# Probabilities times values grouped by head, at slots 2, 5, 8 and 11 of the pair loop

## What is computed

```python
mask = q_bucket[:, :, :, None] == k_bucket[:, :, None, :]
scores = scale * np.matmul(q, k.transpose(0, 1, 3, 2))
scores = np.where(mask, scores, -1000000000.0)
scores = scores - np.max(scores, axis=-1, keepdims=True)
attn = np.exp(scores)
attn = attn / (np.sum(attn, axis=-1, keepdims=True) + 1e-09)
return np.matmul(attn, v).astype(np.float32)
...
X = np.fft.fft(x, axis=1)
X = np.fft.fft(X, axis=2)
```

## Time and profile before

| | us |
|---|---|
| median of three runs | 653.95 (653.85 to 654.36) |
| the profiled execution | 655.48, of which its span 653.7 |
| PE busy in the span | 624.0 |
| VectorE, ScalarE, GpSimd busy | 351.7, 314.6, 245.6 |
| one pair in the loop | 30.01 |

### The profile page before, as it was taken

The page is one execution under the profiler, slowest core; times in us unless marked ns, Lnnn a source line. Parts: engine busy times, 40 slices in busy tenths (PEclk is TensorE's granted clock), DMA queues, the critical chain, the costliest instruction groups (busy, mean ns, idle before and its releaser), DMA issues.

```text
span 653.7 us, 11131 instructions
## 1 busy us (share of the span) xinstructions
PE 624.0 (95%) x3730; PEld 503.3 (77%) x3730; DVE 351.7 (54%) x587; ACT 314.6 (48%) x608; POOL 245.6 (38%) x199
## 2 busy tenths in 40 slices
PE   2899999999999999888999999999999999999998
PEld 1667676667667675887788888888888888888786
DVE  2878797868787785987211111114533333329920
ACT  2777686768686764364422222225333333354242
POOL 6543333333252340845332223334644444313140
PEclk9999999999999999999999999999999999999999
DMA  5822231313242000100122222341212222000102
GB/s 129 249 80 72 73 95 50 96 51 99 70 116 73 1 26 1 50 0 1 34 66 64 64 64 64 121 136 33 71 58 64 64 64 65 16 0 1 76 21 97
DMA packets 34262, 42.08 MB, mean 64 GB/s; under 512 B 3520, under 2 KB 22208, under 8 KB 34240
## 3 DMA queue, kind: packets, MB, share of 16 engines
q1 hardware_dynamic: 32512, 37.77, 19.5%
q0 software_dynamic: 1728, 4.02, 2.2%
HBM read 38.63 MB, written 3.15 MB: 64 GB/s over the span
## 4 chain that ended last, share of the span: by engine, by line
PE 81%; DVE 10%; issue 4%; ACT 2%; POOL 2%; DMA 1%; SPq 0%; ACTq 0%; DVEq 0%; POOLq 0%
PE banks L1487 21%; PE banks L1475 20%; PE banks L1302 10%; PE banks L1285 10%; PE banks L1349 7%; PE banks L1582 4%; DVE row_min L953 2%; PE banks L1241 2%; PE banks L1566 2%; PE banks L1422 2%; DVE x_then_u_then_gate L1160 1%; DVE probT L341 1%; DVE k_b L946 1%; PE banks L1325 1%; POOL row_sums_and_differences L523 1%
## 5 line engine op out<-in xcount | busy, mean ns | idle before, releaser
L1147 DVE SCALAR_TENSOR_TENSOR h_lo<-banks,h_hi 128x512 fp32r<-128x512 f32 x64 | 35.3, 557 | 181.3 <-ACT h_hi L808 181.3
L953 DVE TENSOR_REDUCE row_min<-banks 128x1 f32<-128x768 f32 x96 | 91.2, 955 | 42.2 <-PE banks L1285 41.7
L660 ACT ACTIVATE prob<-banks,row_min 128x768 f32<-128x768 f32 x96 | 87.1, 907 | 31.1 <-DVE row_min L953 31.1
L1475 PE MATMUL banks<-unT_hi,w_hi 128*128 128x512 f32 (+1 forms) x256 | 86.5, 338 | 0.2 <-DVE h_lo L1147 0.2
L1475 PE MATMUL banks<-unT_hi,w_lo 128*128 128x512 f32 (+1 forms) x256 | 86.3, 337 | 0.0
L1475 PE MATMUL banks<-unT_lo,w_hi 128*128 128x512 f32 (+1 forms) x256 | 86.2, 337 | 0.0
L1349 PE MATMUL banks<-ident,prob 128*128 128x128 f32 x576 | 79.6, 273 | 2.4 <-DVE probT L341 1.5
L546 POOL TENSOR_TENSOR w_lo<-w_stage,w_hi 128x512 fp32r<-128x512 f32 x32 | 45.3, 1416 | 80.0 <-ACT w_hi L725 80.0
L484 POOL TENSOR_TENSOR k_b<-k_raw,k_a 64x768 fp32r<-64x768 f32 x16 | 29.1, 1820 | 122.1 <-ACT k_a L643 122.1
L1349 PEld LDWEIGHTS banks<-ident,prob 128*128 128x128 f32 x576 | 67.3, 140 | 9.8 <-ACT probT L341 2.6
L551 POOL TENSOR_TENSOR w_lo<-w_stage,w_hi 128x512 fp32r<-128x512 f32 x32 | 42.2, 1318 | 75.5 <-ACT w_hi L730 75.5
(11 more groups left out here) (147 smaller groups left out, 1192.3 us busy)
## 6 DMA issues: line engine op xcount, KB each, us to landing
w_stage<-in_moe_w_ch SPq DMA_DIRECT2D x64, 256.0 KB, 2.8
q_raw<-in_q SPq DMA_DIRECT2D x32, 192.0 KB, 3.2
k_raw<-in_k SPq DMA_DIRECT2D x32, 192.0 KB, 3.6
v_in<-in_v SPq DMA_DIRECT2D x16, 192.0 KB, 2.4
out<-y_out SPq DMA_DIRECT2D x12, 256.0 KB, 2.0
seq_tables_sb<-in_dft POOLq DMA_DIRECT2D x6, 386.0 KB, 3.5
wvo_stage<-in_moe_w_val SPq DMA_DIRECT2D x1, 1024.0 KB, 5.3
wvo_stage<-in_moe_w_out SPq DMA_DIRECT2D x1, 1024.0 KB, 7.7
```

The source lines that it names most:

```text
L660: act.activation(prob[s % 2][:, :, :], s_tile(s), ACT.Exp, bias=row_min[:, s:s + 1], scale=-1.0, accum_out=row_sum[:, s:s + 1]).then_inc(e ...
L953: dve.tensor_reduce(row_min[:, s:s + 1], s_tile(s), AX.XY, ALU.min).then_inc(min_ready, 1)
L1147: dve.scalar_tensor_tensor(out=h_lo[:, slot, at:at + size], in0=h_bank[c], scalar=0.0, in1=h_hi[:, slot, at:at + size].bitcast(F32), op0=A ...
L1475: op = pe.matmul(h_bank[c], w_[:, slot, kb, :], x_[:, kb, at:at + size], start=(kb == 0 and m == 0), stop=(kb == KB - 1 and m == 2))
```

## The change

The products are grouped by head instead of by half of the queries: a result bank now holds one head, its first 384 queries on partitions 0 to 63 and the others on 64 to 127, and both column halves of PE hold that head's values. Head 0 is multiplied in slots 8 and 11 of its own pair, head 1 in slots 2 and 5 of the next. O moves from slots 3 and 6 to 3 and 9, B from 1 and 7 to 0 and 6. The outT copies go before the exponential of slots 1 and 7, and `round_q` with `copy_q` after that of slots 2 and 8. The values are loaded head by head with a semaphore each. The inverted row sums are held per head, and `write_x` writes 64 columns of all six row tiles instead of 128 columns of three. The first roundings of the folded rows move from slots 0 and 2 to 2 and 3 of pair 8. Pair 1 is written out too, and the loops cover pairs 2 to 6.

```diff
-        PREPARE = {1: ["B"], 2: ["C0"], 4: ["C1"], 7: ["B"], 8: ["C0"], 10: ["C1"]}
+        PREPARE = {0: ["B"], 2: ["C0"], 4: ["C1"], 6: ["B"], 8: ["C0"], 10: ["C1"]}
...
-        OUT_SLOT = {3: 0, 6: 1}
+        OUT_SLOT = {3: 0, 9: 1}
...
-        PV_SLOTS = {11: (0, 0), 1: (0, 1), 2: (1, 0), 4: (1, 1)}
+        PV_PARTS = 2
+        PV_SLOTS = {8: (0, 0, 0), 11: (0, 0, 1), 2: (1, 1, 0), 5: (1, 1, 1)}
...
-            def load_v(i):
-
-                need(sp, pv_done, 2 * i)
-                for h in range(2):
-                    sp.dma_start(v_in[:, h, :, :], v_v[2 * i + h]).then_inc(v_loaded, 16)
+            def load_v(i, h):
+
+                need(sp, pv_done, 2 * i + (h - 1) if not isinstance(i, int) or i else 0)
+                sp.dma_start(v_in[:, h, :, :], v_v[2 * i + h]).then_inc(v_loaded[h], 16)
...
-                    if last == 2 and s in (0, 2):
-                        round_parts(0, s // 2)
                     h, nxt = head_of(s)
                     if s % 6 == 0 and last + nxt < 2:
                         round_k(i + nxt, h)
+                    if s % 6 == 1 and not (isinstance(i, int) and i == 0):
+                        copy_outT(i, s // 6)
                     if last < 2:
                         softmax_exp(i, s)
-                    if s % 6 == 0 and last + nxt < 2:
+                    if s % 6 == 2 and last + nxt < 2:
                         round_q(i + nxt, h)
-                    if s % 6 == 1 and last + nxt < 2:
                         copy_q(i + nxt, h)
-                    if s == 1 and not (isinstance(i, int) and i == 0):
-                        copy_outT(i, 0)
-                    if s == 4 and not (isinstance(i, int) and i == 0):
-                        copy_outT(i, 1)
+                    if last == 2 and s in (2, 3):
+                        round_parts(0, s - 2)
...
-                for kt in range(HT * part, HT * part + HT):
-                    for h in range(2):
-                        op = pe.matmul(PS[h * D:(h + 1) * D, 7, 0:HALF], v_in[:, h, kt, :],
+                for kt in range(T // PV_PARTS * part, T // PV_PARTS * (part + 1)):
+                    for g in range(2):
+                        op = pe.matmul(PS[g * D:(g + 1) * D, 7, 0:HALF], v_in[:, h, kt, :],
                                        probT[h][:, kt, g * HALF:(g + 1) * HALF], start=(kt == 0), stop=(kt == T - 1))
...
-                    if s == 10 and last < 2:
+                    if s == 8 and last < 2:
                         invert_sums(i, 0)
-                    if s == 1 and not first:
+                    if s == 2 and not first:
                         invert_sums(i - 1, 1)
```

More of the change, by code:

```diff
@@ L174, in attention_fft_ffn_gate_kernel @@
         qk_loaded = [sem(f"qk_loaded{h}") for h in range(2)]
-        v_loaded = sem("v_loaded")
+        v_loaded = [sem(f"v_loaded{h}") for h in range(2)]
         scratch_full = [sem(f"scratch_full{r}") for r in range(3)]
@@ L265, in attention_fft_ffn_gate_kernel @@
             counts[-1, (0, task)] = count[n % 3]
-        for i in (0, NP - 1, NP):
+        for i in (0, 1, NP - 1, NP):
             if i == NP - 1:
-                after_first = list(count)
-                count = [c + per * (NP - 2) for c, per in zip(count, PER)]
+                after_second = list(count)
+                count = [c + per * (NP - 3) for c, per in zip(count, PER)]
             for use in uses:
@@ L334, in drain_prob @@
             wait_filled(eng, i, use)
-            if h == 0 and qt % HT == 0:
-                need(eng, pv_done, pair_ * 2 + (qt // HT - 1))
+            if qt == 0:
+                need(eng, pv_done, pair_ * 2 + (h - 1))
             half = int(task[1])
@@ L414, in _ @@
             load_qk(0, 1)
-            load_v(0)
+            load_v(0, 0)
+            load_v(0, 1)
             load_qk(1, 0)
@@ L667, in copy_outT @@
                 if not (isinstance(i, int) and i == 1 and g == 0):
-                    j, use = (i - 1, (6, "O")) if g == 0 else (i, (3, "O"))
+                    j, use = (i - 1, (9, "O")) if g == 0 else (i, (3, "O"))
                     wait_drained(act, j, use)
@@ L715, in _ @@
             pair(0, 0)
-            with act.Fori(1, NP - 1) as i:
+            pair(1, 0)
+            with act.Fori(2, NP - 1) as i:
                 pair(i, 0)
@@ L953, in row_minimum, with invert_sums, write_x @@
                 dve.tensor_reduce(row_min[:, s:s + 1], s_tile(s), AX.XY, ALU.min).then_inc(min_ready, 1)
[L955 to L964, removed]
+            def invert_sums(i, h):
+                need(dve, exp_done, i * SLOTS + T * (h + 1))
+                sums = row_sum[:, T * h:T * (h + 1)]
+                dve.tensor_scalar(row_den[:, h, :], sums, 1e-9, None, ALU.add).then_inc(inv_step, 1)
+                need(dve, inv_step, i * 4 + (2 * h + 1))
+                dve.reciprocal(row_inv[:, h, :], row_den[:, h, :]).then_inc(inv_step, 1)
+            def write_x(i, use, h):
                 j = i - 1
                 wait_filled(dve, i, use)
[L968 to L972, removed]
[L973 to L975 removed]
+                need(dve, inv_step, j * 4 + (2 * h + 2))
+                at = (j % PPB) * P + h * D
+                cols = slice(at, at + D) if isinstance(j, int) else bass.ds(at, D)
+                dve.tensor_tensor(X[:, j // PPB, :, cols].rearrange("p (g t) d -> p t g d", g=2),
+                                  scratch(i, use).rearrange("p (t g d) -> p t g d", t=HT, g=2),
+                                  row_inv[:, h, :].rearrange("p (g t) -> p t g", g=2).unsqueeze(3)
+                                  .broadcast_to([P, HT, 2, D]),
                                   ALU.mult).then_inc(scratch_free[bank_of(i, use)], 1)
@@ L1027, in _ @@
             pair(0, 0)
-            with dve.Fori(1, NP - 1) as i:
+            pair(1, 0)
+            with dve.Fori(2, NP - 1) as i:
                 pair(i, 0)
@@ L1287, in scores, with p_times_v @@
                 op.then_inc(scores_done, 1)
-            def p_times_v(i, g, part):
+            def p_times_v(i, h, part):
                 if part == 0:
-                    tile = T + HT * (g + 1) - 1
+                    tile = T * h + T - 1
                     j, s = (i, tile + 2) if tile + 2 < SLOTS else (i + 1, tile + 2 - SLOTS)
@@ L1361, in pair @@
                     if s in PV_SLOTS:
-                        g, part = PV_SLOTS[s]
-                        if s == SLOTS - 1:
-                            if last < 2:
-                                p_times_v(i, g, part)
-                        elif not first:
-                            p_times_v(i - 1, g, part)
+                        back, h, part = PV_SLOTS[s]
+                        if not back and last < 2:
+                            p_times_v(i, h, part)
+                        if back and not first:
+                            p_times_v(i - 1, h, part)
             pe.wait_ge(consts_ready, 7)
@@ L1374, in _ @@
             pair(0, 0)
-            with pe.Fori(1, NP - 1) as i:
+            pair(1, 0)
+            with pe.Fori(2, NP - 1) as i:
                 pair(i, 0)
```

29 lines of the change are left out of this document (14 added, 15 removed).

## The result

The changed kernel takes 647.69 us, median of four runs (646.75 to 648.04), beside 654.15 (653.85 to 654.78) for the one before on the same chip: ratio 0.9894, interval 0.9882 to 0.9906, or 6.5 us less. The forecast was 648.6, within 647.0 to 652.3. Its direction, its main place and about its size came true; two of its terms were off by 0.8 and 2.2 us in opposite directions, and part of the cause it gave for the old wait is wrong, as the experiments show. That the two misses partly cancel is luck.

What follows compares the result with a forecast made beforehand. TensorE, busy 95% of the span, was taken to wait about 1.02 us per loop pair. Terms +0.6 (first pair), -4.9 (loop), +0.4 (pair 7), -1.4 (tail) gave -5.3 us: 648.6 from 653.95, range 647.0 to 652.3.

Steps and rivals of the forecast that it cites:

- The loop: Pairs 1 to 6: spreading the products removes PE's wait, each pair going from 30.01 to 29.2 us, -4.9 us in all.
- The extra width change: Loop: the new spacing changes the TensorE tile width once more per pair, costing 0.16 us.
- The ring: Loop: scores, row_min, exp, then scores two slots on take 3.13 us, against 3.0 to 3.1 of PE work uncovered.
- That backlog is the 1.02: Slots 5 to 10: VectorE wants 11.9 us against 10.2 of PE work, which makes PE wait 1.02 per pair.
- The thin places: Slots 4 and 5 of each half: banks and drains come with margins of 0.0 and 0.1 us; no wait taken.
- A: Loop rival, half comes back: a narrow margin is late by 0.25 in each half, 3.0 us back, 651.6; chance 0.24.
- First pair: Pair 0 now holds a PV in slot 8 and earlier bits: +0.6 us, between 0 and 2.09.
- Pair 7: Second half lacks preparations, slot 10's drain late for slot 11 by about 1.3 us: +0.4, between 0 and 0.8.
- Tail: After the last twelve transposes: one PV of 2.09 less, outT copy waits of 0.75 and 0.67: -1.4 us.
- GpSimd, SyncE and ScalarE: Moved roundings, outT copies, splits and value loads hide behind other work: cost 0.
- Rival C: All PVs: column halves sharing one head's values no longer overlap, PV takes twice as long, about 715 us; chance 0.05.
- B: Loop rival: the waits only move to slots 3/4 and 0/1, all 4.9 us come back, 653.5; chance 0.07.

Runs made afterwards that it cites:

- the three runs made from it: Kernel before with ScalarE draining both halves in slot 7 (654.80), with copy_q cut to 8 columns from pair 1 on (654.77), or with both (654.85).
- The shifted spacing: Changed kernel with the products still three slots apart but one slot later (9, 0, 3, 6): 672.81, ratio 1.0267 to the kernel before.
- the cut copy without the drain: Kernel before with copy_q cut to 8 columns from pair 1 on, slot 7's drain left as it was: 654.77, ratio 1.0001.
- the last experiment: Changed kernel with later sequence products, pair 0's roundings in their old slots, and pair 7's VectorE folds after the slot's drain: 646.07, ratio 0.9864.
- the two other placings of the products: Changed kernel with products together in slots 10, 11, 4, 5 (665.44, ratio 1.0161), or in slots 9, 0, 3, 6 (672.81, ratio 1.0267).
- the first experiment: Changed kernel with the roundings of q back in slots 0 and 6 (round_q), 1 and 7 (copy_q): 648.20, ratio 0.9901 to the kernel before.

## Why the prediction was right, and where it was off

**The loop, forecast -4.9, measured -7.1.** The largest term has the right place and the right sign: no wait is left, VectorE's busy time is nearly as before (23.91 and 24.20). It is too small because my sum for a pair was 29.2 and TensorE needs 28.84. Slot by slot in the second half: slot 7 1.39 and measured 1.37, slot 8 3.83 and 3.80, slot 9 1.70 and 1.70, slot 10 1.74 and 1.61, slot 11 3.64 and 1.46 + 2.09 = 3.55. The two large misses, 0.13 and 0.09, lie around a bucket product: I took 0.35, my upper end, where a plain one costs 0.26 (124.54 to 124.80), and scores right behind it take 0.71 (124.80 to 125.51), not 0.81. The one of this half with another tile width behind it costs 0.35 (119.05 to 119.40). Some 0.4 a pair, six times, is the 2.2. The prediction had set the 0.35 aside for a bucket product with a width change behind it, and used it in slots 4 and 10, where scores follow: with the 0.10 less for scores behind it, that makes most of the 0.4.

The extra width change was priced at 0.16 and is there at about that: 0.17, the transposes of slot 11 before their products taking 0.75 (125.51 to 126.26) and not 0.58. The Trainium skill, "TensorEngine Tiling (Array Packing)", Tiling Modes, Key Properties, has TensorE drain at a change of mode, and gives no price; here it is 0.17 behind transposes and 0.09 behind a bucket product.

**The cause of the old wait** was half right. The ring from scores to scores two slots on, 3.13, is there; the step "That backlog is the 1.02" fails. The kernel before and the three runs made from it all stay at 5.8 from slot 8 to slot 11, and VectorE waits for PE as slot 8 begins, so no backlog stands there. What lengthens the ring is one bucket pair in it. The forecast came true all the same, by luck as far as this step goes, since the products that give VectorE "time to catch up" are those that cover that pair. The shifted spacing shows what the wrong step would have cost elsewhere: by the count of neighbouring slots I expected 648 to 652, and it ran at 672.81.

**The thin places** didn't bind. A's waits after slot 3 are absent from the loop's rows, and giving that drain away changed nothing.

**First pair, forecast +0.6, measured +1.4.** The bounds 0 and 2.09 held; the value was off by 0.8 between the two traces. PE in both traces (changed, then before) up to the first bucket product:

```profile
14.44 0.98 PE L1285 MATMUL banks<-k_a,q_a 128*128 128x384 f32 x2 [2.35 <-DVE k_b L947]
...
18.88 0.84 PE L1285 MATMUL banks<-k_a,q_a 128*128 128x384 f32 x2
...
20.16 0.95 PE L1349 MATMUL banks<-ident,prob 128*128 128x128 f32 x6
20.86 0.42 PE L1247 MATMUL banks<-bits_sb,bucket_codes_sb 128*128 128x384 f32 x1
```

```profile
14.58 0.98 PE L1285 MATMUL banks<-k_a,q_a 128*128 128x384 f32 x2 [2.35 <-DVE k_b L946]
...
18.84 0.62 PE L1285 MATMUL banks<-k_a,q_a 128*128 128x384 f32 x2
...
19.66 0.82 PE L1349 MATMUL banks<-ident,prob 128*128 128x128 f32 x6
20.23 0.42 PE L1247 MATMUL banks<-bits_sb,bucket_codes_sb 128*128 128x384 f32 x1
```

The same products take 6.42 now and 5.65 before, which is 0.77 of the 1.4. It is hardly the change's: in the changed kernel's trace the slow pace of the last section ends at about 20.4, before at about 18.9. Over all traces these products take 5.27 to 6.30 in the old order (four) and 5.06 to 6.53 in the new one (eight), and in both it grows with the end of the slow pace, to within about 0.2. Where it ends at the same moment, 20.19, the old order (6.30, the cut copy without the drain) and the new one (6.29, the last experiment) take the same.

The rest is the change's. From the first bucket product to the last products of the pair are 18.12 to 18.14 in the four traces of the old order and 18.93 in the changed kernel (20.86 to 39.79): about 0.8, where the working had 0.6.

**Pair 7, forecast +0.4, measured +0.1.** The late drain is there as described, at 1.10 (I said 1.3, from 0.65), and the shorter bucket slots pay part of it back: from the products of slot 2 to those of slot 5 are 6.86 (220.34 to 227.20), where my sum makes 7.08.

**Tail, forecast -1.4, measured -1.1.** One group of 2.09 less, and 0.58 for the last outT copy (0.67 expected). The mis-sized part is ahead of the first group: PE waits twice, 0.33 + 0.70 = 1.03, where I had 0.75. The 0.33 is for ScalarE's drain of the first six transposes, a wait that the prediction did not have. The 0.70 is put down to VectorE's drain, done at 246.74, but the first outT copy is done at 246.69, so the two end together.

**GpSimd, SyncE and ScalarE, forecast 0.** PE waits for none of them in the loop. **Rival C** fell with the 2.09 for a group: two column halves that hold the same head's values overlap as two heads' did. **B** (moved waits, no gain) is wrong here, yet the two other placings of the products did worse than that.

## What to carry to other kernels

Where engines run in step, don't look for the busiest one: follow one chain from a product over the next engine's queue, in its order, back to the product that needs it, and compare its length with the first engine's work in between. Put the long independent work of the first engine exactly there; an even spacing that misses the spot cost 17.5 us here against the kernel before. And where such a chain binds, taking load off an engine outside the chain is worth nothing, while moving one small job behind the one that is waited for brought most of its price (0.76 of 0.87).

## What was not expected of the hardware

At the start TensorE goes at a slower pace, and the windows don't show it. The changed kernel and the one before (length, busy per engine, granted clock, DMA):

```profile
14.44:18.84 4.40, 4.40 (x16) 2.73 (x17) 1.51 (x2) 0.99 (x2) 1.30 (x1) 1.00 0.32 92
```

```profile
14.58:18.84 4.26, 4.26 (x16) 2.59 (x16) 1.91 (x2) 1.61 (x4) 1.30 (x1) 1.00 0.26 76
```

Both say 1.00, but one slot's scores take 1.41 there (14.58 to 15.99 before) and 0.81 in the loop. This 1.00 is not a reading. The trace's record of the granted clock begins only at 18.88 before and at 20.41 in the changed kernel, with an entry at 1.00 (2.4 GHz), and the windows count time without an entry as full. The slow pace ends at these moments: before, the scores that start at 18.84 are the first at full pace, in the changed kernel the bucket product at 20.86. In the first experiment the record begins at 17.69 and full pace at 17.73. Over the fourteen traces it begins between 17.69 and 20.80, late and early ones in both orders. What sets the moment they don't show, and the start of the kernel varies by over 1 us with it.

And the feature stage behind the fold, the same in all kernels, ran with a granted clock that differs between executions. Two stretches of the kernel before and one of the changed kernel:

```profile
291.95:295.36 3.41, 3.41 (x18) 3.37 (x17) 2.50 (x8) 0.96 (x2) 0.95 (x2) 0.50 0.00 0
309.02:312.43 3.41, 3.13 (x14) 2.73 (x15) 2.23 (x8) 2.08 (x4) 1.20 (x4) 0.50 0.00 0
```

```profile
303.72:307.13 3.41, 3.10 (x15) 2.23 (x14) 2.18 (x4) 2.57 (x6) 0.00 (x0) 0.50 0.00 0
```

In these the clock stands at the lower level, 1.2 GHz; all else of that stage is at 1.00 up to the last us of the span. In the first of them the products of 258 columns start 0.21 apart (294.15, 294.36, 294.58), right behind it 0.12 (296.46, 296.59, 296.70). Before it fell, PE had been idle for 1.73 (up to 290.29). Of twelve traces (all but the two slow placings), three have no such stretch in the stage, five have one and four have two. From the fold's start to the end of the span they take 391.0 to 391.1, 391.6 to 392.1 and 392.1 to 392.7, with either order among those with one and with two. The changed kernel's trace has one (391.6 = 646.0 - 254.43), the trace before two (392.7 = 653.7 - 261.05), and that is the 1.1 by which their spans differ beyond the fold. A span from one profile thus varies by up to 1.7 us here without the change; the moment of the fold is better for a change that lies ahead of it.
